# Attention with two expert layers on one core: how x of the expert tiles is loaded and made, and when the expert pieces begin

## What is computed

```python
scores = scale * np.matmul(q, k.transpose(0, 1, 3, 2))
thresh = np.max(scores, axis=-1, keepdims=True) - tau
scores = np.where(scores >= thresh, scores, -1000000000.0)
attn = softmax(scores)                      # written out in the reference
attn_out = np.matmul(attn, v)
x = attn_out.transpose(0, 2, 1, 3).reshape(2304, 512)
h = x @ w_in                                # first layer
x = (h * np.clip(h + 3.0, 0.0, 6.0) / 6.0) @ w_out
h = x @ w_in2                               # second layer
return (h * (1.0 / (1.0 + np.exp(-1.702 * h)))) @ w_out2
```

## Time and profile before

| | us |
|---|---|
| median of 3 executions | 1161.23 (1159.36 to 1161.65) |
| the profiled execution | 1159.2 |
| its span, first to last instruction | 1157.4 |
| TensorE busy | 1093.3 (94%) |
| VectorE busy | 560.6 (48%) |
| ScalarE busy | 550.1 (48%) |
| GpSimd busy | 490.9 (42%) |

### The profile page before, as it was taken

The page is one execution under the profiler, slowest core; times in us unless marked ns, Lnnn a source line. Parts: engine busy times, 40 slices in busy tenths (PEclk is TensorE's granted clock), DMA queues, the critical chain, the costliest instruction groups (busy, mean ns, idle before and its releaser), DMA issues.

```text
span 1157.4 us, 17664 instructions
## 1 busy us (share of the span) xinstructions
PE 1093.3 (94%) x6720; PEld 1027.0 (89%) x6720; DVE 560.6 (48%) x1038; ACT 550.1 (48%) x1034; POOL 490.9 (42%) x582
## 2 busy tenths in 40 slices
PE   4888799999999999878999999999999999999998
PEld 3767599999999989878999999999999999999997
DVE  3889788778877887224322222232222223222221
ACT  4788686867676776235423333333233223332221
POOL 3466655455645563268333332243333222222222
PEclk9999899999999999989999999999999999999999
DMA  3445563256335522454333211222221002222210
GB/s 109 120 129 151 137 143 103 77 134 169 89 93 134 144 74 77 114 139 141 112 119 118 88 60 54 83 91 91 92 91 55 28 28 82 83 82 82 82 55 27
DMA packets 90627, 112.36 MB, mean 97 GB/s; under 512 B 25120, under 2 KB 69296, under 8 KB 90544
## 3 DMA queue, kind: packets, MB, share of 16 engines
q1 hardware_dynamic: 90544, 111.25, 33.3%
HBM read 78.12 MB, written 33.10 MB: 96 GB/s over the span
## 4 chain that ended last, share of the span: by engine, by line
PE 82%; DVE 6%; issue 4%; ACT 4%; POOL 2%; DMA 1%; SPq 0%; ACTq 0%; POOLq 0%; DVEq 0%
PE mm L489 19%; PE score L500 17%; PE tr L489 13%; PE score L498 10%; PE score L451 7%; PE tr L466 6%; PE mm L480 5%; PE mm L498 5%; DVE prob L598 2%; DVE neg_max L590 2%; DVE pt_lo L616 1%; POOL w_lo L884 1%; ACT gate L749 1%; POOL g_lo L894 1%; DMA inv_b<-inv_scratch 1%
## 5 line engine op out<-in xcount | busy, mean ns | idle before, releaser
L894 POOL TENSOR_TENSOR g_lo<-act_f,g_hi 128x384 fp32r<-128x384 f32 (+1 forms) x208 | 197.7, 955 | 421.5 <-ACT g_hi L757 421.5
L489 PE MATMUL mm<-x_hi,w_hi 128*128 128x384 f32 (+1 forms) x512 | 163.7, 320 | 7.9 <-DVE x_lo L622 7.9
L489 PE MATMUL mm<-x_hi,w_lo 128*128 128x384 f32 (+1 forms) x512 | 162.8, 318 | 0.0
L489 PE MATMUL mm<-x_lo,w_hi 128*128 128x384 f32 (+1 forms) x512 | 162.7, 318 | 0.0
L725 ACT ACTIVATE pt_hi<-tr 128x640 fp32r<-128x640 f32 x144 | 101.7, 706 | 96.5 <-PE tr L466 95.7
L752 ACT ACTIVATE gate<-mm 128x384 f32<-128x384 f32 x48 | 23.6, 492 | 220.5 <-PE mm L489 220.5
L451 PE MATMUL score<-k_hi,q_sp 128*128 128x288 f32 x320 | 98.8, 324 | 29.9 <-DVE prob L598 18.6
L616 DVE TENSOR_TENSOR pt_lo<-tr,pt_hi 128x640 fp32r<-128x640 f32 x144 | 118.3, 821 | 16.2 <-ACT pt_hi L725 14.9
L590 DVE TENSOR_REDUCE neg_max<-score 128x1 f32<-128x576 f32 x144 | 108.2, 751 | 31.1 <-PE score L451 28.3
L867 POOL TENSOR_SCALAR thresh<-neg_max,tau_abs 128x1 f32<-128x1 f32 x144 | 42.0, 292 | 186.3 <-DVE neg_max L590 185.4
L466 PE MATMUL tr<-ident,prob 128*128 128x128 f32 x720 | 106.9, 281 | 14.7 <-issue 12.3
(11 more groups left out here) (73 smaller groups left out, 2439.8 us busy)
## 6 DMA issues: line engine op xcount, KB each, us to landing
x_raw<-x_t_scratch SPq DMA_DIRECT2D x18, 768.0 KB, 6.2
q_raw<-in_qT SPq DMA_DIRECT2D x64, 144.0 KB, 2.9
k_raw<-in_kT SPq DMA_DIRECT2D x64, 144.0 KB, 2.8
stage<-in_w_in SPq DMA_DIRECT2D x16, 512.0 KB, 6.8
stage<-in_w_out SPq DMA_DIRECT2D x16, 512.0 KB, 7.1
o_parts_scratch<-o_t SPq DMA_DIRECT2D x32, 160.0 KB, 1.8
x_raw<-o_parts_scratch SPq DMA_DIRECT2D x16, 288.0 KB, 5.3
part<-o_parts_scratch SPq DMA_DIRECT2D x16, 288.0 KB, 6.2
```

What stands on the lines that cost most here:

```text
L489: m = pe.matmul(bank[:, 0:width], w[:, col:col + P], x[:, k, 0:width], start=(k == 0 and e == 0), stop=(k == KC - 1 and e == 2))
L894: pool.tensor_tensor(g_lo[:, c, 0:width], act_f[:, c % 2, 0:width], g_hi[:, c, 0:width], ALU.subtract).then_inc(g_lo_done, 1)
```

## The change

The six DMAs of a tile's x become twelve, three for each chunk, and chunk k is loaded, made and split in slots of its own. In even tiles (also tile 6) chunks 0 to 2 are loaded 10, 7 and 4 slots ahead of the start of the next batch, each right behind the attention of its pair, and chunk 3 is loaded 3 slots after the start. The makes stand at -7, -4, -1 and +6, the splits at 0, 1, 2 and +7. In odd tiles the chunks are loaded one by one beside the pieces 1, 3, 5 and 7 of the tile before. GpSimd waits for the chunk it makes (`chunk_loaded[k]`, three DMAs), no longer for all of x. Pieces begin at slot 36b + 8. So the last piece stands in slot 152, and one piece less lies behind slot 143. Piece 0 waits for 14 quarters of w_lo, those of w_in among them; the first y piece waits for all 16. In the rest of the mixed part tile 7 is loaded in twelve DMAs too. The tensor `o_parts` has its two parts as a dimension of its own.

```diff
+    LAG = 8
...
-        g0, every = BATCH_SLOTS * b + SLOTS + 1, 8 if b + 1 < B else 6
+        g0, every = BATCH_SLOTS * b + LAG, 8 if b + 1 < B else 6
...
-        at = END - 8 if ti == MIXED else AT[ti, 0] - 5 if ti % 2 == 0 else AT[ti - 1, 9]
+        after = BATCH_SLOTS * (ti // 2 + 1)
         for k in range(KC):
-            MAKE_X[at + k], SPLIT_X[at + k + 1] = (ti, k), (ti, k)
+            if ti % 2 == 0:
+                slots = after + (-10, -7, -4, 3)[k], after + (-7, -4, -1, 6)[k], after + (0, 1, 2, 7)[k]
+            else:
+                slots = AT[ti - 1, 2 * k + 1], AT[ti - 1, 9] + k, AT[ti - 1, 9] + k + 1
+            for table, g in zip((LOAD_X, MAKE_X, SPLIT_X), slots):
+                table[g] = (ti, k)
...
+            def load_chunk(ti, k):
+
+                _, t0, width = TILES[ti]
+                batch, col = divmod(t0, S)
+                i = KC * batch + k
+                wait(sp, x_lo_done, KC * (ti - 1) + k + 1)
+                wait(sp, x1_stored, 16 * ti)
+                sp.wait_ge(inv_stored[i % 2], 16 * (i // 2 + 1))
+                sp.wait_ge(o_stored[0], 16 * (2 * i + 2))
+                sp.wait_ge(o_stored[1], 16 * (2 * i + (2 if col else 1)))
+                cols = slice(col, col + width)
+                sp.dma_start(x_raw[:, k, 0:width], o_parts[2 * i:2 * i + 2, 0, :, cols]).then_inc(chunk_loaded[k], 16)
+                sp.dma_start(x_low[:, k, 0:width], o_parts[2 * i:2 * i + 2, 1, :, cols]).then_inc(chunk_loaded[k], 16)
+                inv = inv_t[i, cols]
+                sp.dma_start(inv_b[:, k, :], bass.AP(tensor=inv.tensor, offset=inv.offset,
+                                                     ap=[[S, 2], [0, HD], list(inv.ap[0])])).then_inc(chunk_loaded[k], 16)
...
-                if g % BATCH_SLOTS == 2 and g > 2:
-                    load_x(2 * (g // BATCH_SLOTS - 1))
+                if g in LOAD_X:
+                    load_chunk(*LOAD_X[g])
                 if g in MAKE_X and MAKE_X[g][1] == KC - 1:
                     store_x(MAKE_X[g][0])
-                piece = PIECE.get(g)
-                if piece is not None and piece[0] % 2 == 0 and piece[1] == 3:
-                    load_x(piece[0] + 1)
...
-                        pe.wait_ge(w_lo_done, 4 * UNITS)
+                        pe.wait_ge(w_lo_done, 4 * UNITS - 2)
...
+                if p == FC:
+                    pe.wait_ge(w_lo_done, 4 * UNITS)
...
-                if k == 0:
-                    pool.wait_ge(x_loaded, loads_x(ti))
-                    wait(pool, x_lo_done, KC * ti)
+                pool.wait_ge(chunk_loaded[k], 48 * (ti + 1))
```

More of the change, by code:

```diff
@@ L80, in attention_moe_kernel @@
     END = max(PIECE) + 2
-    MAKE_X, SPLIT_X = {}, {}
+    LOAD_X, MAKE_X, SPLIT_X = {}, {}, {}
     for ti in range(MIXED + 1):
-        at = END - 8 if ti == MIXED else AT[ti, 0] - 5 if ti % 2 == 0 else AT[ti - 1, 9]
+        after = BATCH_SLOTS * (ti // 2 + 1)
         for k in range(KC):
-            MAKE_X[at + k], SPLIT_X[at + k + 1] = (ti, k), (ti, k)
+            if ti % 2 == 0:
[4 more added lines that the diff above has]
+                table[g] = (ti, k)
     MIX_ITEMS = FC + KC
-    o_parts = nc.dram_tensor("o_parts_scratch", (NH, 2 * HD, S), F32).ap()
+    o_parts = nc.dram_tensor("o_parts_scratch", (NH, 2, HD, S), F32).ap()
     inv_t = nc.dram_tensor("inv_scratch", (PAIRS, SLOTS * P), F32).ap()
@@ L196, in attention_moe_kernel @@
         inv_stored = [sem(f"inv_stored{i}") for i in range(2)]
+        chunk_loaded = [sem(f"chunk_loaded{k}") for k in range(KC)]
         x_loaded = sem("x_loaded")
@@ L255, in first_item @@
             return sum(FC + blocks_y(t) for t in range(MIXED, ti))
-        def loads_x(ti):
-            first = FIRST[1]
-            return 16 * (6 * min(ti + 1, first) + max(ti + 1 - first, 0))
         def y_part(buffer, ti, m):
@@ L293, in store_group @@
                 wait(sp, o_copied, n + 1)
-                sp.dma_start(o_parts[h, :, col:col + width], o_t[:, n % 2, 0:width]).then_inc(o_stored[n % 2], 16)
+                sp.dma_start(o_parts[h, :, :, col:col + width], o_t[:, n % 2, 0:width]).then_inc(o_stored[n % 2], 16)
             def store_inverse(i):
@@ L322, in load_x @@
             def load_x(ti):
                 step, t0, width = TILES[ti]
[L324 to L346, removed]
+                sp.wait_ge(x_lo_done, KC * ti)
@@ L348, in store_x @@
+                sp.dma_start(x_raw[:, :, 0:width], PLAN[step][0][:, t0:t0 + width].rearrange("(k p) n -> p k n", p=P)
+                             ).then_inc(x_loaded, 16)
             def store_x(ti):
@@ L411, in _ @@
                         sp.wait_ge(y_stored, 16 * ti)
-                    load_x(ti + 1)
+                    if ti == MIXED:
+                        for k in range(KC):
+                            load_chunk(ti + 1, k)
+                    else:
+                        load_x(ti + 1)
                 t = ti - FIRST[step]
@@ L742, in high_x @@
                 elif k == 0:
-                    act.wait_ge(x_loaded, loads_x(ti))
+                    act.wait_ge(x_loaded, 16 * (ti - FIRST[1] + 1))
                 act.activation(x_hi[:, k, 0:width], x_raw[:, k, 0:width], ACT.Copy).then_inc(x_hi_done, 1)
```

## The result

The changed kernel takes 1231.62 us (1230.34 to 1234.69), the kernel before 1161.44 beside it: a ratio of 1.061 (1.058 to 1.064), 70 us slower where 17 us less were forecast. The profiled execution has a span of 1230.0 us.

The account below looks back on a forecast made before the run. TensorE, busy 94%, was taken as the bound, so its idle and low-clock stretches could give time. +1.9 - 6.4 - 2.4 - 7.9 - 1.6 - 0.8 = -17.2 us gave 1144.0 us as a median; range 1139.0 to 1150.0.

Parts of the forecast that it names:

- part d: Stop before tile 6: last chunk loads in 5.5 us behind pieces; 7.93 us stop goes, plus 1.6 us of lower clock.
- part b: TensorE's hole in batch 1, mask 43 to mask 48: 16.2 us instead of 22.57, 6.4 us less.
- first rival: Before tile 6, its last chunk is late all the same; typical 1147 us, at most 1150.5; chance 0.14.
- part a: Tile 0's x earlier: three splits moved into slots that VectorE bounds, costing 1.9 us; GpSimd's extra work costs nothing.
- part f: Other tiles' loads as 12 DMAs in slots TensorE bounds: taken as 0, with up to 4 us of gain possible.
- T: End of pt_lo's product in slot 145, 474.49 us before; the load of tile 6's last chunk is timed from it.
- third rival: SyncE's one row: chunk loads hold up q, k, v loads and o_t stores; 1172 us at 1 us each; chance 0.03.
- What the profile would show: Signs of right or wrong; wrong included ScalarE's v_hl waiting for v_raw and tile 6's first matmul waiting for x_lo.
- the prediction's alternative: Tile 0's splits, moved away from the makes, cost some 1.2 us, making the sum 0.7 us better.
- c: Two pieces done early: 1.58 us behind the last attention slot, 0.84 us in a slot before 143; together 2.4 us.
- e: TensorE's idle 0.81 us before the product at 475.30, a wait for o_t's copy, goes behind piece 25.

Follow-up runs that it names:

- e1_halves: Changed kernel with every chunk DMA cut into two of 64 partitions, 72 KB each; 1140.74 us, ratio 0.984 to the kernel before.
- m1_shapes: Kernel before plus six 144 KB probe loads, one at a time, only the source's outermost count differing; counts 2, 4, 8, 16: 5.58, 3.74, 3.09, 2.63 us.
- e9_merged: Changed kernel with o_parts laid out so a head pair's rows lie at one distance, the inverse in halves, more stores; 1141.61 us, ratio 0.982.
- e8_wait16: e1_halves with piece 0 waiting for all 16 quarters of w_lo; 1143.90 us, ratio 0.984.
- e7b_lag10: e1_halves with pieces beginning 10 slots behind a batch and the splits of tile 6 two slots later; 1143.06 us, ratio 0.985.
- e1_again: The same kernel as e1_halves, measured again beside e8_wait16; 1140.85 us, ratio 0.982.
- m2_behind: Kernel before plus probes: three loads with outermost count 2 and one 128-row load behind, 12.8 us; all four with 128 single rows, 5.3 us.
- e2_before_pairs: Kernel before with twelve loads of 2 x 64 rows per tile at the old place; 1382.79 us, ratio 1.193.
- m3_more_shapes: Kernel before plus nine probes of other load shapes and of stores, one at a time; stores with 2, 8, 128 outermost: 5.38, 2.82, 1.78 us.

## Why the prediction was wrong, point by point

**The step that failed** is the price of a chunk's load. In part d I bounded it by 4.2 and 7.2 us, from loads whose sources are 64 rows (q, and the six x loads), and in part b I took it to be "3 x 144 KB, a quarter of what stood in v's way". The bounds came from rows of another shape. "No row here shows 144 KB from this scratch" stood in the text, in the first rival, and I let the byte count fill that gap. Parts a and f put the same loads at nothing, part f because their issue would lie beside TensorE's work: a for three chunks of tile 0 beside the attention, f for all tiles between. What they cost, measured against e1_halves, is 16.5 us up to mask 43 (it starts at 144.98, 18.8 us later than before, where part a had 1.9), 48.0 from there to mask 142, where part f had 0, and 26.5 behind it. From mask 43 to mask 48 the changed kernel takes 20.3 us, where part b had 16.2.

In part d T is 531.41 in the changed kernel, and the last chunk of tile 6 was landed 12.5 us after its first issue, where I had 5.5 (the chain, issue and landing of its last load, and a last load of tile 7):

```profile
534.77 0.51 SPq L335
...
535.87 11.41 DMA inv_b<-inv_scratch
...
580.51 13.25 DMA inv_b<-inv_scratch
```

x_lo of tile 6 ends at 549.98, T + 18.6, where I had T + 11.6 and at most T + 13.3, and TensorE waits 6.46 us for it. Tile 7 in its turn is loaded with too little to hide it: the landing of a last load takes up to 13.25 us, and TensorE's first matmul there waits 16.3 us.

**The first rival** named this late chunk, at T + 17.5 if it took as long as all the bytes of before. It came even later, by the number of DMA engines and not by the bytes, and its price of at most 6.5 us is the small part of the loss. Its estimate of 2.3 us per load rests on a figure that the Trainium skill gives for DMAs issued by GpSimd, while SyncE issues these; m1_shapes shows 2.5 to 2.6 us for this size with 16 or more outermost, and 5.58 with 2.

**The rule that I missed** speaks against this change, and a page of the Trainium skill has it (above). I weighed the advice to coalesce small transfers instead, which says nothing of this. Another rule of the Trainium skill, DMA: Bandwidth & Descriptors, section "Rules for kernel authors", to use one transfer over 128 partitions rather than two over halves, is what the change does; in this kernel the halves win by 91 us, because joining them put a 2 outermost. Where the rows join (e9_merged), one transfer is as good as two halves, 1141.6 against 1140.9 us, and no better. The measurement decides.

**The third rival** had the right place (v behind the x loads in SyncE's row, ScalarE waiting) and a chance of 0.03. Its mechanism was issue time at 0.62 us; the real one is an issue that is held up for 2 to 3 us. Its price of 1 us per chunk would have given 1172; e1_halves against the changed kernel gives 91/32 = 2.8 us per chunk. So that it pointed the right way is in part luck. "What the profile would show" has this wait among its signs of being wrong, and it is what the trace shows.

**The sum, tested on e1_halves.** With the shape repaired the time is 1140.7, inside the range, 3.3 below the forecast. Its masks (timeline of VectorE) and the end of the mixed part:

```profile
128.52 0.81 DVE L603 SCALAR_TENSOR_TENSOR prob<-score,thresh,prob 128x576 f32<-128x576 f32 x1
```

```profile
128.52:145.46 16.94, 15.28 (x111) 14.08 (x110) 13.66 (x29) 12.83 (x25) 10.67 (x14) 1.00 0.52 141
```

```profile
479.29 3.41 PE mm L492 x24
```

- Part a: mask 43 starts at 128.52, 2.33 us later than in the earlier trace rows; forecast 1.9. The amount is close by luck. Against the kernel before the three splits add 0.8, nothing and 1.1 us: two of them take less than the mean of 0.64 (0.46 and 0.44), as the prediction's alternative had it, and the third 0.72, but the first and the third wait some 0.6 us for x_hi, and the second hides. The other half microsecond is no split at all. VectorE's small operation behind the totals takes 0.74 us where it took 0.16, while a make runs on GpSimd (110.23 to 111.90); that the make causes it is not shown. These are the lines of that operation in e1_halves and in the kernel before, and that of the third split:

```profile
110.31 0.74 DVE L610 TENSOR_SCALAR total_e<-total 128x9 f32<-128x9 f32 x1
```

```profile
110.41 0.16 DVE L605 TENSOR_SCALAR total_e<-total 128x9 f32<-128x9 f32 x1
```

```profile
120.08 0.72 DVE L627 TENSOR_TENSOR x_lo<-x_raw,x_hi 128x288 fp32r<-128x288 f32 x1 [0.59 <-ACT x_hi L749]
```

- Part b: from mask 43 to mask 48 16.94 us; forecast 16.2, before 22.57. Right to 0.7 us, and the clock is 1.00 there. The loosened wait belongs to this part and is no further term: 3.0 us instead of about 1 (e8_wait16).
- Parts c and f up to mask 142: 310.1 us after mask 48, before 313.1: 3.1 us less, where c had 0.8 and f had 0. e7b_lag10, with the pieces at their old place, has 310.8 (143.42 to 454.21). So the earlier pieces gave 0.7 and part f was worth 2.3 us of the 4 that its upper bound allowed; I should not have taken nothing where a range has a plain reason for a gain.
- Parts c and e behind mask 142: to the end of the pieces 23.7 us, before 27.5: 3.8; forecast 2.4.
- Part d: with T at 466.92, x_lo of tile 6 ends at 479.14, T + 12.2, and tile 6 starts at 479.29, T + 12.4, where I had T + 11.6 for x and T + 12.4 for the pieces. The stop is 0.11 us instead of 7.93, without anything to spare. The first 24 matmuls take 3.41 us; forecast 3.16.

These add up to 19.4 us up to there, and 18.4 less of span are left at the end. The 1.0 us between is lost in one stretch behind a wait of TensorE for GpSimd's g_lo: from 526.00 to 531.00 the granted clock is 0.52, in the same work before (545.30 to 550.30) 0.72, and in e1_again (526.00 to 531.00) 0.77. The forecast had 17.2. That it is so close is partly luck, since a and b came out 1.2 us worse, c, e and f together 3.7 better, and 1.0 was lost later.

## What to carry to other kernels

Before a DMA is priced by its bytes, look at the outermost dimension of its DRAM side as it is built: blocks of rows that don't join at one distance put the number of blocks there, and a small number confines the whole transfer to that many DMA engines (2, 4 and 8 in m1_shapes). What is issued behind it has parts on the same engines and waits for them (m2_behind). A price bound taken from rows must come from rows of the same shape; where none exists, that is an unknown with no upper end, and a rival with a real chance. A low DMA share together with issues that take 3 us is how this looks in a profile, and in e2_before_pairs it made the kernel 222 us slower without more bytes.

## What the runs showed of the hardware that I had not expected

- A load of 128 rows of 1152 bytes takes 5.58 us with 2 outermost, 3.74 with 4, 3.09 with 8, about 2.6 from 16 on (m1_shapes); a store 5.38 with 2, 2.82 with 8, 1.78 with 128 (m3_more_shapes). One DMA engine takes 0.054 us per such row, worked out from the first and the last of these loads.
- Slow loads behind each other use the same two engines (m2_behind): one goes out about every 3.2 us from the fourth on in e2_before_pairs, and SyncE's issue of the v load that comes next takes as long, 3.12 us.
- The cost grows faster than the number of slow loads: 7, 25 and 90 us for one, two and three per chunk. Even one is not free.
